# Moving the product with V of two heads ahead of the next head's transposes, from the mixed tile on

## What is computed

```python
B, H, S, D = q.shape                       # 2, 8, 576, 64
scores = scale * np.matmul(q, k.transpose(0, 1, 3, 2))
kth = np.partition(scores, -top_k, axis=-1)[..., -top_k:-top_k + 1]      # top_k = 32
scores = np.where(scores >= kth, scores, -1000000000.0)
attn = softmax(scores)                     # with 1e-09 added to the sum
x = np.matmul(attn, v)                     # -> (B * S, H * D) = (1152, 512)
...
P = sinkhorn(x @ w_gate)                   # 8 rounds
out = sum(P[:, e:e + 1] * (np.maximum(x @ w1[e], 0.0) @ w2[e]) for e in range(8))
h = out @ w_in
return (h * np.tanh(softplus(h))) @ w_out
```

## Time and profile before

| | |
|---|---|
| median of 3 runs | 1239.48 us (1239.37 to 1240.28) |
| the profiled execution | 1242.88 us |
| its span, first to last instruction | 1241.0 us |
| PE busy | 1198.6 us (97%) |
| DVE busy | 899.6 us (72%) |
| ACT busy | 687.6 us (55%) |
| POOL busy | 642.6 us (52%) |

### The profile page before, as it was taken

How to read it: one execution, slowest core, us unless ns; L and a number is a source line. 1 busy time by engine, 2 the same in 40 slices (tenths; PEclk the granted TensorE clock), 3 DMA queues, 4 the chain that set the end, 5 groups by cost and what they waited for, 6 DMA issues and landing times.

```text
span 1241.0 us, 19573 instructions
## 1 busy us (share of the span) xinstructions
PE 1198.6 (97%) x6676; PEld 1071.3 (86%) x6676; DVE 899.6 (72%) x1556; ACT 687.6 (55%) x1226; POOL 642.6 (52%) x393
## 2 busy tenths in 40 slices
PE   4878999999999999999999999999999999999998
PEld 4777889999999998999888999999888888898777
DVE  6989998899999971446646564646464647887886
ACT  5666776767777664442243333333333337888776
POOL 1857965555656567763376666666666630000000
PEclk8599999999999999999999999999999999999999
DMA  9023432233323233332233222222222122222230
GB/s 170 9 86 120 144 104 93 94 94 107 110 90 111 86 111 102 120 102 93 85 106 107 69 75 76 75 80 74 86 67 94 52 68 85 69 69 84 86 125 36
DMA packets 150486, 112.10 MB, mean 90 GB/s; under 512 B 34832, under 2 KB 124944, under 8 KB 150416
## 3 DMA queue, kind: packets, MB, share of 16 engines
q1 hardware_dynamic: 150416, 111.19, 29.6%
HBM read 104.09 MB, written 7.08 MB: 90 GB/s over the span
## 4 chain that ended last, share of the span: by engine, by line
PE 86%; DVE 7%; ACT 3%; POOL 2%; issue 2%; DMA 1%; SPq 0%; ACTq 0%; DVEq 0%; POOLq 0%
PE ps L903 16%; PE ps L728 15%; PE ps L741 15%; PE ps L964 14%; PE ps L1031 7%; PE ps L1087 7%; PE ps L637 4%; PE ps L608 3%; DVE top L1486 2%; DVE work L1488 2%; PE ps L618 2%; PE ps L597 1%; POOL s_sb L1961 1%; PE ps L632 1%; POOL e_sb L1964 1%
## 5 line engine op out<-in xcount | busy, mean ns | idle before, releaser
L1890 POOL TENSOR_TENSOR w_lo<-w_raw,w_hi 128x1024 fp32r<-128x1024 f32 x90 | 219.6, 2440 | 114.4 <-ACT w_hi L1114 114.3
L1114 ACT ACTIVATE w_hi<-w_raw 128x1024 fp32r<-128x1024 f32 (+1 forms) x172 | 179.4, 1044 | 0.6 <-DMA w_raw<-in_k 0.6
L1486 DVE MAX8 top<-work 128x8 f32<-128x576 f32 x216 | 152.3, 747 | 0.0
L728 PE MATMUL ps<-x_hi,w_hi 128*128 128x384 f32 (+3 forms) x384 | 128.2, 334 | 0.1
L728 PE MATMUL ps<-x_hi,w_lo 128*128 128x384 f32 (+3 forms) x384 | 127.4, 332 | 0.0
L728 PE MATMUL ps<-x_lo,w_hi 128*128 128x384 f32 (+3 forms) x384 | 127.2, 331 | 0.0
L1897 POOL TENSOR_TENSOR ha_lo<-h_f,ha_hi 128x384 fp32r<-128x384 f32 (+1 forms) x72 | 72.0, 999 | 90.4 <-ACT ha_hi L1191 90.4
L903 PE MATMUL ps<-w_hi,h_lo 128*128 128x512 f32 x296 | 117.1, 396 | 0.0
L903 PE MATMUL ps<-w_lo,h_hi 128*128 128x512 f32 x296 | 116.9, 395 | 0.0
L903 PE MATMUL ps<-w_hi,h_hi 128*128 128x512 f32 x296 | 115.3, 390 | 0.0
L1488 DVE MATCH_REPLACE8 work<-top,work 128x576 f32<-128x576 f32 x144 | 105.9, 743 | 0.0
(11 more groups left out here) (185 smaller groups left out, 3273.1 us busy)
## 6 DMA issues: line engine op xcount, KB each, us to landing
w_raw<-in_moe_w SPq DMA_DIRECT2D x288, 256.0 KB, 3.0
w_raw<-in_moe_w_in SPq DMA_DIRECT2D x32, 256.0 KB, 2.8
w_raw<-in_moe_w_out SPq DMA_DIRECT2D x32, 256.0 KB, 3.1
spill<-y_out SPq DMA_DIRECT2D x5, 768.0 KB, 3.8
y_in<-spill SPq DMA_DIRECT2D x5, 768.0 KB, 4.4
q_parts<-in_q SPq DMA_DIRECT2D x18, 128.0 KB, 3.3
vones<-in_v SPq DMA_DIRECT2D x8, 256.0 KB, 4.9
out<-acc SPq DMA_DIRECT2D x8, 256.0 KB, 2.7
```

Source lines behind the costliest of these rows:

```text
L728: last = nc.tensor.matmul(ps[:, bank, 0:w], wt[:, s, 0, c * P:(c + 1) * P], xt[:, c, token:token + w], start=(n == 0), stop=(n == len(term ...
L1114: return nc.scalar.activation(dst, src, ACT.Copy)
L1486: last = v_.max(top[:, b, op // 2, :], src)
L1890: g_.tensor_tensor(w_lo[:, s, :, :].rearrange("p a n -> p (a n)"), w_raw[:, s, :, :].rearrange("p a n -> p (a n)"), w_hi[:, s, :, :].rearr ...
```

## The change

In tiles from the mixed one on, PE no longer makes the product in the odd head, between `up_a` and `down_before`. It makes it at the start of the even head that follows, ahead of that head's transposes; the last one of a tile (heads 2 and 3) thus stands in head 0 of the next tile, and behind the last tile it has a line of its own. ACT's copy of it moves likewise. In head 7 the transposes of x get a wait of their own for ACT's copies, since both use one bank of PSUM. In Pool's program `chunk_a` is taken apart: in head 3 the queries' low part comes between its halves, and in even heads `pair_done`, a wait for DVE's mask of the odd head whose even partner PE transposes in this head, stands ahead of the weights' half.

```diff
--- before.py
+++ after.py
@@ -624,6 +624,7 @@
 
             def attend(T, h, parts):
 
+
                 if h % 2 == 0:
                     return
                 pe.wait_ge(o_copied, head(T, h - 1) + FREE)
@@ -666,6 +667,8 @@
                     if first and h == 4:
                         pe.wait_ge(q_copied, 4)
                         pe.wait_ge(k_copied, KEYS_0)
+                    if not early and h % 2 == 0 and (h > 0 or not isinstance(T, int) or T > MIX):
+                        attend(T - 1 if h <= 4 else T, (h - 5) % H, before if h <= 4 else parts)
                     if late_parts is not None:
                         probs_transposed(late, (h - 4) % H)
                     scores(T, h, parts)
@@ -683,9 +686,10 @@
                     if first and h == 4:
                         pe.wait_ge(v_ones, 2)
                         pe.wait_ge(v_in[0], 16 * V_LOADS)
-                    if late_parts is not None:
+                    if early and late_parts is not None:
                         attend(late, (h - 4) % H, late_parts)
                     if not early and h == H - 1:
+                        pe.wait_ge(pt_copied, head(T, h - 4) + 1 + FREE)
                         x_transposed(T - 1)
                     if expert is not None:
                         down_before(expert, f)
@@ -828,6 +832,7 @@
                 down_before(n // NF, n % NF)
 
             pe.wait_ge(x_copied, NT - 1)
+            attend(NT - 1, 3, FULL1)
             for h in range(4, H):
                 probs_transposed(NT - 1, h)
                 next_chunk(AFTER - H + h, lambda: attend(NT - 1, h, FULL1))
@@ -1218,6 +1223,8 @@
                 for h in range(H):
                     late, late_on = (T - 1, before) if h < 4 else (T, True)
                     expert, f = chunk_at(T, h)
+                    if not early and h % 2 == 0 and (h > 0 or not isinstance(T, int) or T > MIX):
+                        output_copied(T - 1 if h <= 4 else T, (h - 5) % H)
                     if late_on:
                         probs_copied(late, (h - 4) % H)
                     scores_copied(T, h, late_on)
@@ -1231,7 +1238,7 @@
                         queries_copied(T, h + 2)
                     if h in (5, 6) and following:
                         queries_copied(T + 1, h - 5)
-                    if late_on:
+                    if early and late_on:
                         output_copied(late, (h - 4) % H, two_before if h < 4 else before)
                     if h == (4 if first else 3) and following:
                         queries_high(T + 1)
@@ -1284,6 +1291,7 @@
                 between()
                 after_chunk(n // NF, n % NF)
 
+            output_copied(NT - 1, 3)
             for h in range(4, H):
                 probs_copied(NT - 1, h)
                 if h < 6:
@@ -1941,6 +1949,12 @@
                 up_lo(*after)
                 sums_lo(*after)
 
+            def pair_done(T, h):
+
+
+                late = T - 1 if h < 4 else T
+                pool.wait_ge(topk, topk_value(late, (h - 4) % H + 1, MASKED))
+
             def tile_with_chunks(T, following=True):
 
                 for h in range(H):
@@ -1948,9 +1962,13 @@
                         normalised(T - 1, 0)
                     if h == H - 1:
                         normalised(T - 1, 1)
-                    chunk_a(*chunk_at(T, h))
+                    expert, f = chunk_at(T, h)
+                    hidden_low(expert, f)
                     if h == 3 and following:
                         queries_low(T + 1)
+                    if h % 2 == 0:
+                        pair_done(T, h)
+                    split_lo(A0 + expert * NF + f + AHEAD, (f + AHEAD) % RING)
                 x_low(T - 1)
 
             def mask(T, h):
```

## The result

| | before | after |
|---|---|---|
| median of 19 runs | 1239.59 us (1238.79 to 1242.82) | 1241.94 us (1240.67 to 1246.79) |
| ratio | | 1.0020, 95% interval 1.0013 to 1.0026 |
| profiled span | 1241.0 us | 1239.1 us |

The change costs 0.2%, between 1.6 and 3.2 us by the interval. The forecast was +1.0 us with a range that holds the result, and it called that "no change"; it lies on the edge between that and "slower".

A forecast was written before the change was run, and what follows sets the result against it. The prediction took PE's instructions to bound the kernel: -1.0 us from the moved products and +2.0 us from PE's wait for x gave +1.0 us on 1239.48, so 1240.5 us, range 1238.0 to 1243.7.

The forecast's parts named there:

- PE is the bound, DVE is not: Steady tile: PE's instructions set its 51.72 us; DVE's fullness is partly masks stretched by Pool, with 3.4 us to spare.
- The product saves 0.20 us a tile: Product with V, moved ahead of even heads' transposes, costs PE 1.95 us each; 1.0 us saved over five tiles.
- x is asked for 0.5 us too early, in tiles 5 to 8: Head 7: PE waits for Pool's x before transposing it, 0.5 us a tile, 2.0 us in all; nothing in tile 4.
- Pool's waits are met: Pool's four added waits on masks are met before Pool gets there: cost 0, nothing gained.
- ACT and the added wait on PE cost nothing: ACT's moved product copy and PE's wait in head 7 for ACT's four-heads-old copies: cost 0 each.
- Sum: Whole kernel: -1.0 + 2.0 = +1.0 us on the 1239.48 us median, 1240.5 us, called "no change".
- Rival A: Head 7: x is never late, so the 2.0 us wait goes and the saving stays: 1238.5 us; chance 0.14.
- Rival B: Head 7: x comes behind both masks, wait 1.3 us a tile, +4.2 us: 1243.7 us, slower; chance 0.15.
- Rival C: Even heads: Pool's splits run behind colliding masks, x gets late, PE waits 2.5 us more in head 7: 1250; chance 0.04.
- Rival D: Moved products: their matmuls today hide waits of 0.25 us or more each, 20 give 5 us: 1236.5 us; chance 0.10.

The follow-up runs named there:

- Run 7: Changed kernel, Pool normalising x's second half in head 6 and waiting in even heads on the next pair's masks, which its split meets; ratio to before 0.9994.
- run 1: Changed kernel, with Pool normalising the second half of x in head 6, ahead of its splits, instead of head 7; ratio to the kernel before 0.9993.
- run 5: Changed kernel, with the product of heads 2 and 3 put back in head 7 ahead of x's transposes; ratio to the kernel before 0.9996.
- run 3: Changed kernel, with Pool's program as before: no wait on masks, queries' low part behind the weights; ratio to the kernel before 1.0009.
- run 4: Kernel before, with only Pool's part of the change: waits on masks, queries' low part ahead of the weights; ratio to the kernel before 1.0007.
- run 6: Changed kernel, with Pool normalising the second half of x behind head 7's hidden part, not ahead of it; ratio to the kernel before 1.0147.

## Why the prediction was right, and where its sizes were off

- *PE is the bound, DVE is not.* Right. Run 7 took 6 us a tile from DVE and the tile stayed.
- *The product saves 0.20 us a tile.* The mechanism was right, the size too large: a steady tile is 51.57 to 51.59 us without the wait, a saving of 0.13 to 0.15. Heads 3 and 5 give up 0.06 us each (head 3 was priced at 0.08 by a difference of heads). What was missed is that the even heads get about 0.01 us longer, with the product ahead of their transposes (head 4 takes 5.14 to 5.15 us for 5.13). In all 0.7 us, not 1.0.
- *x is asked for 0.5 us too early, in tiles 5 to 8.* Right, term by term: the split at +5.66 us (forecast 5.65), the transposes 0.46 us late (0.46), 0.66 us long, nothing in tile 4. The four tiles together pay 2.1 us (2.0 forecast), and runs 1 and 5 took that away.
- *Pool's waits are met.* Right, as far as runs 3 and 4 can show. *ACT and the added wait on PE cost nothing.* No run shows a cost.
- *Sum.* +1.0 was forecast, the trace shows +1.4: 0.3 of the 0.4 is the saving that was sized too large, 0.1 the wait. The median shows +2.4, within the range, but on the border of what was called "slower" (2.5), to which the forecast gave a chance of 0.23; one microsecond of it no term of the sum explains, and it was luck that it didn't cross the border. Near such a border the chances should have been more even: a sum of +1.0 with a wait that is paid in full wherever it grows leans to one side.
- *Rival A* claimed that masks are tied to the end of the split in every steady tile. That didn't hold for head 0: once PE has waited, DVE is ahead, and its first mask there starts before the split and makes the split wait. In head 7, where it counts, it held.
- *Rival B*: x was served between the masks, not behind both. *Rival C*: run 7 built it with x early, which takes away its price; with x in head 7 it was not built, and its 10 us stay an estimate. That masks and splits wait for each other is shown: run 7 has masks of 0.80 to 0.82 us once no split meets them, and the split that starts behind a mask takes 3.00 us for 2.40. The Trainium skill (SBUF — State Buffer, "SBUF: two separate sides") has the shared port pair taken by whichever of GpSimd and a DVE operation with two SBUF inputs starts first, for the whole instruction, and these traces agree. *Rival D* didn't come: no run shows a saving beyond 0.7 us.

## What to carry to other kernels

When work is moved off a place on the bounding engine, look at what it covered there: here the product of heads 2 and 3 gained nothing by moving and stood in front of a consumer whose input came 0.7 us too late for the new place, and still 0.46 after Pool had moved up. An engine that shows 100% beside another at 100% may be stretched by waits that the profile counts as busy; compare the shortest and the longest of its equal instructions. And a wait that is written into a program to keep two operations apart must be on the operation that it collides with: here it named the pair before, and did nothing.

## What the runs showed of the hardware

An idle time of 2.6 us on PE was followed by a fall of the granted clock from 1.00 to 0.50 in some tiles and not in others (tiles 6 and 7 of run 6, with the same wait), at 6.6 / 4 = 1.65 us on average. The waits of 0.3 us in the changed kernel left it at 1.00 (tiles 5 to 8). So a stall of a few microseconds on PE has a price that differs from one occurrence to the next.

Masks that wait for Pool's split are counted as busy: 3.62 us for a pair that takes 1.6 free. It goes the other way too: a split that started 0.06 us behind a mask was counted as busy for 3.00 us instead of 2.40. Both before and after, the two engines were served in the order of asking around head 7 of tile 6: split, first mask, x, second mask. In the changed kernel the first mask ended at 336.46, x at 336.93, and the second mask took 1.06 us for a free 0.82.
